# Last two layers in groups of four tiles, first transform by row tiles, and the gate logits of the last head pair one step later

## The chip, the cores and the metric

The kernel runs on one core of a Trainium2 chip. The metric is the device time of one launch in microseconds. In the profile PE is TensorE (PEld its weight loads), DVE is VectorE, ACT is ScalarE, POOL is GpSimd, and SP is the sync engine, which here only issues DMAs.

## What is computed

Three blocks in a row on 2 x 768 tokens of width 512, all in float32:

```python
# 1. attention: a window of +-15 keys plus 24 block summaries, 8 heads of 64
scores_all = np.concatenate([scores_l_m, scores_s], axis=-1)
a = softmax(scores_all);  out = a @ np.concatenate([v, v_sum], axis=2)
# 2. mixture of 8 experts, token by token; the expert is carried over while a local gate is >= 0.5
logits = x @ w_gate;  local_gate = sigmoid(x @ w_local)
e = argmax(logits[s]) if s == 0 or local_gate[s] < 0.5 else prev_e
out[s] = p[e] * (np.maximum(x[s] @ w1[e], 0) @ w2[e])
# 3. Fourier mixing over sequence and features, then two dense layers
u = x + np.real(fft2(x))
un = (u - mu) / np.sqrt(var + 1e-6)
y = u + np.maximum(un @ w_ch1, 0) @ w_ch2      # w_ch1 is 512 x 2048, w_ch2 2048 x 512
```

## The kernel before

Each engine has its own hand-written instruction stream, and semaphores tie them together. 128 tokens are a tile; there are 12 tiles, 6 of each batch (`ST` = 6, `NT` = 12).

**Attention** works through 8 pairs-of-heads steps in which `attend` handles the 6 tiles `t` of a pair: probabilities turned on PE (L1722), scores (L1713), values (L1736 to 1738). The tables `GATE_TURN`, `GATE_SUM` and `BEHIND` say beside which `(pair, t)` PE turns a tile's activations (`turn_gate`, L1745), ACT copies them to `mid` (`gate_rows`, L736), PE forms the 9 logits (`logits`, L1753) and DVE fetches them (`fetch_logits`, L990). In the last pair the logits of tile 6 stand at t = 3 and those of tiles 7 and 8 behind the values of t = 4 and 5; those of tiles 9 to 11 come after attention. Then PE turns the first 128 sorted rows (`turn_rows(0, 0)`, L1839), keeps busy with six unused matmuls (`unread`, L1882), and starts the first expert layer.

**Experts**: rows sorted by expert in steps of 128; every step has `first_layer` (L1851, 24 matmuls), `turn_rows` of the next step, `second_layer` of the previous one (L1876, 24 matmuls) and `turn_hidden` (L1863). Matmuls are exact splits of float32 in three products of rounded parts (high x high, low x high, high x low); ACT makes the high part and DVE subtracts for the low one (L1392). Four steps are written out and 18 stand in a loop with a test on the number in use (13 steps in this data); skipped ones cost only their tests. The last `second_layer(used - 1)` stands behind the loop. DVE scales the result (L1500), POOL scatters it to DRAM (`folded_y`, L593), SP waits for all of that and gathers the rows back (L492), one DMA for a row tile and its mirror.

**Transform**: DVE folds each gathered pair of row tiles in an even (L1528 to 1532) and an odd half (L1534 to 1543); `fold(b)` makes all three evens of a batch and then all three odds. PE first runs 40 unused matmuls (L2016), then `along_sequence(b)`: for each output chunk the sum over the three row tiles, two cosine chunks and one column (L1938 with a closing row L1940) and two sine chunks (L1951), in plain float32, which the trace counts as two matmuls each. `along_features` follows (L1962 to 1971), DVE and POOL add the results to natural and mirrored rows.

**Last two layers**: `GT` = 3 tiles form a group of `GN` = 384 tokens, in `GROUPS` = 4 groups: 0 and 2 are the natural halves of a batch, 1 and 3 the mirrored ones. A unit `F` is one of 16 chunks `f` of 128 hidden channels for one group: `first` is 12 matmuls of 384 columns into bank 2 or 3 (L1998), ACT takes relu (L885), DVE the low part (L1646), and `second` is 9 matmuls of 512 columns into banks 4 to 6 (L2011). PE does `first(F + 1)` ahead of `second(F)`. In every unit ACT and DVE also split the next 128 columns of `w_ch1` (L851, L1392) and rows of `w_ch2` (L856, L1392), since the weights are kept only as read. The activations of the next group are turned in four chunks during a group (`turn_centred`, L1988; `TURN_AT`). Mean and variance of all tiles are taken in group 0's units, and ACT takes the square root in unit 13 (`deviations`, L840). At the end of a group `finish` (L1614) scales the 3 banks and adds the residual; SP stores natural tiles (L505), POOL mirrored ones with an indirect DMA (L651). The four groups are a loop of two steps of two groups.

## Time and profile before

| | |
|---|---|
| time, three runs | 667.31 us median (666.71, 667.31, 671.98) |
| the profiled execution | 672.55 us, of which its span is 670.6 us |
| mean granted PE clock of it | 0.973 of full speed |
| busy | PE 625.5 us, DVE 364.0, ACT 270.8, POOL 129.2 |
| chain of work that ended last, by engine | PE 79%, DVE 6%, issue 4%, DMA 3%, ACT 3% |
| chain, costliest lines | L2011 20%, L1998 18%, L1876 10%, L1851 9% |
| stages of the span, by the timeline | attention to about 133 us, experts to 319.5, transform 319.5 to 384.9, last layers 384.9 to 659.8, stores and end to 670.6 |

The profile is of one execution of the program; its times are microseconds from the span's start. A chain row is a piece of work on the path that ended last; idle time of an engine off that path costs nothing.

### The profile page before, as it was taken

Reading aid. Unit: us, or ns where it says so; the run is one execution under the profiler, and the core shown is the slowest. Engines: PE = TensorE matmul, PEld = TensorE weight load, DVE = VectorE, ACT = ScalarE, POOL = GpSimd, SP = SyncE. Lnnn points to the kernel's source line nnn. Section 1 sums busy time; section 2 is a strip of 40 time slices with the busy share of each in tenths; the row PEclk is TensorE's granted clock in tenths of the full one; section 3 lists DMA queues with packets and bytes.
Section 4 is the critical chain, followed back from the end, with each engine's and each line's share of the span. In section 5 each row is a group of like instructions: output and inputs, shape, how many; then the busy total and the mean of one; then the engine's idle time right before and its main releaser. Section 6 shows DMA issues by size and latency. Waiting matters only on the chain.

```text
span 670.6 us, 11120 instructions
## 1 busy us (share of the span) xinstructions
PE 625.5 (93%) x3282; PEld 531.4 (79%) x3283; DVE 364.0 (54%) x956; ACT 270.8 (40%) x593; POOL 129.2 (19%) x155
## 2 busy tenths in 40 slices
PE   4799998899889999998899999999999999999993
PEld 3799998878667888886534589988999899989992
DVE  4788687568472585232451666655444544454441
ACT  3488775445132364111011534453443343433330
POOL 5566544203610010010000412030000310000001
PEclk9999999879999999998979999999999999999997
DMA  6958533694454455310503240001000100010001
GB/s 152 170 125 181 127 77 120 216 323 150 183 195 167 157 162 164 152 63 17 203 0 112 92 173 1 0 1 49 1 0 1 47 0 0 0 47 0 0 0 47
DMA packets 59300, 61.61 MB, mean 92 GB/s; under 512 B 42688, under 2 KB 42816, under 8 KB 58240
## 3 DMA queue, kind: packets, MB, share of 16 engines
q1 hardware_dynamic: 54384, 47.21, 24.0%
...
q14 instruction: 19, 0.16, 0.1%
...
## 4 chain that ended last, share of the span: by engine, by line
PE 79%; DVE 6%; issue 4%; DMA 3%; ACT 3%; SPq 1%; another core or an unknown queue 1%; POOL 1%; DVEq 0%; ACTq 0%; POOLq 0%
PE bank L2011 20%; PE bank L1998 18%; PE bank L1876 10%; PE bank L1851 9%; PE bank L1713 3%; PE bank L1938 2%; PE bank L1753 2%; PE bank L1722 2%; ACT arena L703 1%; PE bank L1839 1%; PE bank L1951 1%; PE bank L1863 1%; PE bank L1962 1%; PE bank L1736 1%; PE bank L1745 1%
## 5 line engine op out<-in xcount | busy, mean ns | idle before, releaser
L1998 PE MATMUL bank<-parts 128*128 128x384 f32 x768 | 146.1, 338 | 2.1 <-DVE parts L1392 2.1
L2011 PE MATMUL bank<-parts 128*128 128x512 f32 x576 | 143.8, 394 | 0.7 <-DVE parts L1646 0.3
L1392 DVE TENSOR_TENSOR parts<-arena,parts 128x512 fp32r<-128x512 f32 (+1 forms) x140 | 98.8, 737 | 83.0 <-ACT parts L856 77.9
L1998 PEld LDWEIGHTS bank<-parts 128*128 128x128 f32 x768 | 135.5, 188 | 7.1 <-DVE parts L1392 2.8
L2011 PEld LDWEIGHTS bank<-parts 128*128 128x128 f32 x576 | 106.7, 188 | 21.7 <-DVE mid L1614 1.3
L1851 PE MATMUL bank<-parts 128*128 128x512 f32 x312 | 77.8, 403 | 3.1 <-issue 2.3
L1876 PE MATMUL bank<-parts 128*128 128x512 f32 x312 | 76.2, 401 | 4.9 <-DVE parts L1392 4.5
L856 ACT ACTIVATE parts<-arena 128x512 fp32r<-128x512 f32 x64 | 40.4, 631 | 82.2 <-PE bank L2011 82.2
L1876 PEld LDWEIGHTS bank<-parts 128*128 128x128 f32 x312 | 58.8, 192 | 17.9 <-issue 3.6
L1851 PEld LDWEIGHTS bank<-parts 128*128 128x128 f32 x312 | 59.0, 193 | 16.5 <-issue 4.5
L1392 DVE TENSOR_TENSOR parts<-bank,parts 128x512 fp32r<-128x512 f32 (+1 forms) x56 | 35.1, 649 | 33.6 <-ACT parts L846 23.5
L885 ACT ACTIVATE parts<-bank 128x384 fp32r<-128x384 f32 x64 | 31.4, 491 | 53.7 <-PE bank L1998 53.7
L1646 DVE SCALAR_TENSOR_TENSOR parts<-bank,parts 128x384 fp32r<-128x384 f32 x64 | 35.6, 556 | 26.2 <-ACT parts L885 26.1
L703 ACT ACTIVATE arena<-arena,small 128x184 f32<-128x184 f32 x96 | 42.1, 440 | 15.3 <-DVE small L948 14.5
L651 POOL DMA_INDIRECT out<-mid,cst x6 | 6.1, 1020 | 203.0 <-DVE mid L1614 202.4
L1713 PE MATMUL bank<-arena 128*128 128x184 f32 x192 | 41.6, 344 | 1.8 <-ACT arena L683 1.3
L851 ACT ACTIVATE parts<-arena 128x512 fp32r<-128x512 f32 x64 | 39.5, 617 | 0.0
L593 POOL DMA_INDIRECT folded_y<-mid,dest_i x13 | 12.7, 978 | 129.6 <-DVE dest_i L1501 129.3
L549 POOL TENSOR_TENSOR mid<-mid 128x1024 f32<-128x1024 f32 (+3 forms) x28 | 33.7, 1205 | 12.5 <-DMA mid<-in_v 8.8
L795 ACT ACTIVATE parts<-bank 128x512 fp32r<-128x512 f32 x26 | 14.1, 594 | 51.4 <-PE bank L1863 39.2
L1713 PEld LDWEIGHTS bank<-arena 128*128 128x128 f32 x192 | 32.4, 207 | 3.0 <-ACT arena L683 1.7
L948 DVE CUSTOM_DVE_ANT_0 arena<-bank,cst 128x184 f32<-128x184 f32 x96 | 29.3, 342 | 9.7 <-PE bank L1713 8.8
...
## 6 DMA issues: line engine op xcount, KB each, us to landing
...
```

The costliest lines, as they stand in the source:

```text
L549: pool.tensor_tensor(blocks[:, par, 0:n], blocks[:, par, 0:n], blocks[:, par, n:2 * n], ALU.add).then_inc(halved, 1)
L703: last = act.activation(probs[:, t % 3, (2 * NSP - NS) * hh:(2 * NSP - NS) * hh + NS], masked[:, t % 3, hh, :], ACT.Exp, scale=-1.0, bias= ...
L851: act.activation(m1_hi[:, f % 2, :].rearrange("p (c n) -> p c n", c=DC), m1_raw[:, :, P * f:P * f + P], ACT.Copy).then_inc(m1h_ok, 1)
L856: act.activation(m2_hi[:, f % 2, :], m2_raw[:, f, :], ACT.Copy).then_inc(m2h_ok, 1)
L885: act.activation(g_hi[:, f % 2, :], bank[2 + f % 2][:, 0:GN], ACT.Relu).then_inc(ghi_ok, 1)
L1392: return dve.tensor_tensor(out, whole, upper.bitcast(F32), ALU.subtract)
L1646: dve.scalar_tensor_tensor(g_lo[:, f % 2, :], bank[2 + f % 2][:, 0:GN], 0.0, g_hi[:, f % 2, :].bitcast(F32), ALU.max, ALU.subtract).then_i ...
L1713: last = pe.matmul(S_BANK[t % 2][:, NS * hh:NS * hh + NS], qT[:, par, hh, P * t:P * t + P], k_win[:, par, t, keys], start=True, stop=True)
L1851: last = pe.matmul(bank[1 + half][:, :], x[:, r], w[:, c, f], start=(c == 0 and x is xT_hi and w is w1_hi), stop=(c == DC - 1 and w is w1_lo))
L1876: last = pe.matmul(bank[5][:, :], x[:, c, :], w[:, c // 2, f], start=(c == 0 and x is hT_hi and w is w2_hi), stop=(c == FC - 1 and w is w2 ...
L1998: last = pe.matmul(bank[2 + f % 2][:, 0:GN], w[:, f % 2, r], x[:, par, c, :], start=(c == 0 and w is m1_hi and x is cT_hi), stop=(c == DC ...
L2011: last = pe.matmul(bank[4 + t][:, :], x[:, f % 2, r], w[:, f % 2, :], start=(f == 0 and x is g_hi and w is m2_hi), stop=(f == MC - 1 and w ...
```

## The change

- **Groups of four.** `GT` becomes 4, so `GN` is 512 and there are 3 groups. The tiles are dealt out by a table `TILES`: group 0 takes tiles 0, 3, 1, 4 (two natural tiles of batch 0 and their mirrors), group 1 tiles 5, 9, 10, 11, group 2 tiles 2, 6, 7, 8. `first` has 12 matmuls of 512 columns and `second` 12 of 512, into banks 4 to 7; there are 48 units in place of 64, written out without loops and tests. The next group is turned at units 7, 9, 11, 13. ACT centres four tiles of group 0 and not three, two of them mirrored ones that POOL has to add first.
- **End of a group.** PE signals each finished tile of the last unit (`tile_ps`), and `finish` scales it then; `finish` stands ahead of the turned chunk and of `lower2`. The stores go tile by tile to SP (natural) and POOL (mirrored); the last group has natural tiles only. `out_sb` has its own place in `mid`.
- **Transform.** The first `along_sequence` goes by row tile: for tile j all cosine sums, then all sine sums, in five banks. `fold` makes even and odd of one tile before the next.
- **Last second layer** of the experts stands in the loop, under a test `used < n + 2`; the unused matmuls in front of the transform are 28 and not 40.
- **Gate.** In the last pair the logits are one step later: tile 6 at t = 4, tile 7 at t = 5, tiles 8 to 11 after attention; ACT's copies stay where they were (`GATE_COPY`). `turn_gate` of tiles 10 and 11 waits no longer for the copy ahead, the first sorted rows are turned between the logits of tiles 9 and 10, and the six unused matmuls are gone. DVE has the first two chunks of w1's low part ahead of the rows, and fetches two logits around the split of the rows.

```diff
-GT = 3
+GT = 4
-TURN_AT = {5: (0,), 7: (1,), 9: (2,), 11: (3,)}
+TURN_AT = {7: (0,), 9: (1,), 11: (2,), 13: (3,)}
+TILES = (0, KC, 1, KC + 1) + (KC + 2, ST + KC, ST + KC + 1, ST + KC + 2) + (2, ST, ST + 1, ST + 2)
...
-        BEHIND = {(PAIRS - 1, t): ST + t - 3 for t in (ST - 2, ST - 1)}
+        BEHIND = {(PAIRS - 1, t): ST + t - 4 for t in (ST - 2, ST - 1)}
...
+            for n in NATURAL:
+                sp.wait_ge(o_sb, n + 1 + GT)
+                b, c = TILES[n] // ST, TILES[n] % ST
+                sp.dma_start(out[b, P * c:P * c + P, :], out_sb[:, n % GT, :]).then_inc(natural_out[n % GT], 16)
...
+            fetch_logits(ST + 2)
+            lower_first(w1_lo, w1_raw, w1_hi, w1_hi_ok, w1_lo_ok, 0)
             fetch_logits(ST + 3)
-            lower_first(w1_lo, w1_raw, w1_hi, w1_hi_ok, w1_lo_ok, 0)
-            fetch_logits(ST + 4)
-            fetch_logits(ST + 5)
+            lower_first(w1_lo, w1_raw, w1_hi, w1_hi_ok, w1_lo_ok, 1)
             rows_landed(0)
             dve.tensor_copy(meta_next, xs(0)[:, DM:DM + 2]).then_inc(meta_in, 1)
+            fetch_logits(ST + 4)
             split_x(0)
-            for c in range(1, DC):
+            fetch_logits(ST + 5)
+            for c in range(2, DC):
...
             def fold(b):
                 for c in range(KC):
+                    fold_even(b, c)
+                    fold_odd(b, c)
...
             def finish(g):
-                dve.wait_ge(l2_ps, MC * (g + 1) + TWO)
                 dve.wait_ge(rstd_ok, 1)
                 for c in range(GT):
                     n = GT * g + c
-                    dve.wait_ge(o_free, n + 1)
+                    if c < GT - 1:
+                        dve.wait_ge(tile_ps, (GT - 1) * g + c + 1)
+                    else:
+                        dve.wait_ge(l2_ps, MC * (g + 1) + TWO)
+                    if g:
+                        dve.wait_ge(*stored(n - GT))
...
-            second_layer(used - 1)
+                        with pe.If(used < n + 2):
+                            second_layer(n)
...
+                if b == 0:
+                    for j in range(KC):
+                        pe.wait_ge(even_ok, j + 1)
+                        for o, r, free, n, done in to:
+                            cosines(o, r, j)
...
+                        pe.wait_ge(odd_ok, j + 1)
+                        for c in range(FD):
+                            last = sines(c, j)
...
-            for _ in range(40):
+            for _ in range(28):
                 pe.matmul(bank[7][:, :], xT_hi[:, 0:P], w1_hi[:, 0, 0:512], start=True, stop=True)
```

Two places of PE's order follow. The first is between attention and the experts. `128x9` rows are logits, `cst,x_all 128x128` rows with `xs_first0` turn the sorted rows, other such rows turn a tile for the gate, and `128x256` are the unused matmuls. Before:

```order
L1745 MATMUL bank<-cst,x_all 128x128 [waits xg_sb,att_out]
L1745 MATMUL bank<-cst,x_all 128x128 x3
L1753 MATMUL bank<-cst,mid 128x9 [waits xg_sb,lg_sb]
L1753 MATMUL bank<-cst,mid 128x9 x3
L1753 MATMUL bank<-cst,mid 128x9 [waits xg_sb,pT_sb]
L1753 MATMUL bank<-cst,mid 128x9 x3
L1839 MATMUL bank<-cst,x_all 128x128 [waits xs_first0,lg_sb]
L1839 MATMUL bank<-cst,x_all 128x128 x3
L1882 MATMUL bank<-cst 128x256 x3
L1843 TENSOR_LOAD table_i [waits lg_sb,table_ok]
```

The same place of the change:

```order
L1738 MATMUL bank<-cst,mid 128x9 [waits xg_sb,lg_sb]
L1738 MATMUL bank<-cst,mid 128x9 x3
L1730 MATMUL bank<-cst,x_all 128x128 [waits att_out]
L1730 MATMUL bank<-cst,x_all 128x128 x3
L1822 MATMUL bank<-cst,x_all 128x128 [waits xs_first0,lg_sb]
L1822 MATMUL bank<-cst,x_all 128x128 x3
L1738 MATMUL bank<-cst,mid 128x9 [waits xg_sb,pT_sb]
L1738 MATMUL bank<-cst,mid 128x9 x3
L1738 MATMUL bank<-cst,mid 128x9 [waits xg_sb]
L1738 MATMUL bank<-cst,mid 128x9 x3
L1826 TENSOR_LOAD table_i [waits lg_sb,table_ok]
```

The turned rows moved ahead of the last two sets of logits, the last gate tile is turned behind another set, and the unused matmuls are gone.

The second place is the start of the transform, PE: the unused matmuls, then batch 0 of `along_sequence`. `386` rows are cosine sums (`1x386` the single column, L1940 the closing row), `384` rows sine sums. Before:

```order
L2016 MATMUL bank<-parts 128x512 x40
L1938 MATMUL bank<-arena 128x386 [waits even_ok,yc_sb,tables_in]
L1938 MATMUL bank<-arena 128x386 [waits even_ok] x2
L1940 MATMUL bank<-cst,arena 128x386 [waits row_ok]
L1938 MATMUL bank<-arena 128x386 [waits even_ok,yc_sb]
L1938 MATMUL bank<-arena 128x386 [waits even_ok] x2
L1940 MATMUL bank<-cst,arena 128x386 [waits row_ok]
```

The change:

```order
L2023 MATMUL bank<-parts 128x512 x28
L1918 MATMUL bank<-arena 128x386 [waits ys_sb,z_sb,yc_sb,even_ok,tables_in]
L1918 MATMUL bank<-arena 128x386
L1918 MATMUL bank<-arena 1x386
L1921 MATMUL bank<-arena 128x384 [waits odd_ok]
L1921 MATMUL bank<-arena 128x384
L1918 MATMUL bank<-arena 128x386 [waits even_ok]
```

Five sums of the first row tile now stand ahead of the wait for the second tile; before, each chunk waited for all three tiles in turn.

## Rows read from the trace of the kernel before

**Rows 1.** The page, part 1: busy us (share of the span) x instructions

```profile
PE 625.5 (93%) x3282; PEld 531.4 (79%) x3283; DVE 364.0 (54%) x956; ACT 270.8 (40%) x593; POOL 129.2 (19%) x155
```

**Rows 2.** Chain that ended last (start, us, what): the last layers

```profile
400.34 2.10 PE bank L1998 x12
402.44 2.08 PE bank L2011 x9
...
655.67 4.14 PE bank L2011 x18
```

**Rows 3.** Timeline (start, us, engine line op, [idle before <-releaser]), the last layers

```profile
438.86 0.49 PE L1988 MATMUL bank<-cst,mid 128*128 128x128 f32 x3
...
448.52 2.37 PE L1998 MATMUL bank<-parts 128*128 128x384 f32 x12 [0.79 <-DVE parts L1392]
...
459.53 2.34 PE L2011 MATMUL bank<-parts 128*128 128x512 f32 x9 [0.26 <-DVE mid L1614]
```

**Rows 4.** Timeline of the end

```profile
659.99 2.07 DVE L1614 SCALAR_TENSOR_TENSOR mid<-bank,small,x_all 128x512 f32<-128x512 f32 x3 [3.20 <-PE bank L2011]
...
663.66 0.96 POOL L651 DMA_INDIRECT out<-mid,cst  x1 [0.30 <-issue]
```

**Rows 5.** DMA issues from 590 us on (count, KB each, us to landing)

```profile
out<-mid SPq DMA_DIRECT2D x3, 256.0 KB, 2.1
out<-mid,cst POOLq DMA_INDIRECT x3, 2.7
```

**Rows 6.** Timeline, end of the experts and start of the transform

```profile
310.16 1.29 DVE L1392 TENSOR_TENSOR parts<-bank,parts 128x512 fp32r<-128x512 f32 x2
...
312.09 7.37 PE L1876 MATMUL bank<-parts 128*128 128x512 f32 x24 [2.82 <-DVE parts L1392]
...
319.29 9.23 PE L2016 MATMUL bank<-parts 128*128 128x512 f32 x40
...
327.34 0.69 DVE L1528 TENSOR_TENSOR mid<-x_all 128x512 f32<-128x512 f32 x1 [6.89 <-DMA x_all<-folded_y]
...
328.77 0.89 PE L1938 MATMUL bank<-arena 128*128 128x386 f32 x2 [0.25 <-DVE arena L1532]
...
331.77 0.69 DVE L1528 TENSOR_TENSOR mid<-x_all 128x512 f32<-128x512 f32 x1 [1.80 <-DMA x_all<-folded_y]
```

**Rows 7.** Windows: length, busy PE, PEld, DVE, ACT, POOL, granted clock, DMA share, GB/s

```profile
313.60:317.00 3.40, 3.40 (x10) 2.66 (x9) 0.00 (x0) 0.00 (x0) 0.00 (x0) 0.50 0.00 0
334.10:344.30 10.20, 9.99 (x15) 3.43 (x16) 9.92 (x35) 0.98 (x2) 0.00 (x0) 0.50 0.02 7
344.50:384.00 39.50, 38.29 (x136) 19.85 (x134) 11.04 (x26) 12.21 (x28) 7.48 (x10) 1.00 0.22 80
```

**Rows 8.** Timeline, between attention and the experts

```profile
125.61 1.03 PE L1753 MATMUL bank<-cst,mid 128*128 128x9 f32 x8 [1.03 <-ACT mid L736]
...
131.05 3.67 SPq L445 DMA_DIRECT2D x_all<-sorted_x  x4
...
135.90 3.23 PE L1753 MATMUL bank<-cst,mid 128*128 128x9 f32 x16
...
142.00 4.53 PEld L1851 LDWEIGHTS bank<-parts 128*128 128x128 f32 x18
```

**Rows 9.** Timeline, start of the last layers

```profile
376.51 0.72 ACT L836 ACTIVATE mid<-x_all,small 128x512 f32<-128x512 f32 x1
...
384.88 4.44 PE L1998 MATMUL bank<-parts 128*128 128x384 f32 x24 [1.31 <-DVE parts L1392]
```

**Rows 10.** Chain, `along_sequence` of batch 1: its first and last piece

```profile
349.86 1.95 PE bank L1938 x6
...
358.41 4.09 PE bank L1951 x12
```

**Rows 11.** DMA issues from 117 to 145 us: the sorted rows

```profile
x_all<-sorted_x SPq DMA_DIRECT2D x4, 258.0 KB, 3.2
```

**Rows 12.** Chain, experts: a piece that no engine's row explains

```profile
178.73 4.40 another core or an unknown queue
```

332 lines of the change are left out of this document (153 added, 179 removed).

## The prediction

> **What bounds the kernel now.** I read the page first: PE is busy for 93% of the span [rows 1], so what counts is how fast PE gets through its work and where it is idle or slow. Next the chain of work that ended last: from 384.9 us to 659.8 it is almost only PE, 2.10 us for a `first` (12 matmuls of 384 columns) and 2.08 for a `second` (9 of 512), one behind the other [rows 2]. The timeline of that stretch shows what breaks it [rows 3], and that of the end shows 10.8 us between the last matmul (655.67 + 4.14 = 659.81) and the span's end, of which the last finish, the last indirect DMA and its landing are the larger part [rows 4, 5]. Then the passages between stages: from the last expert step to the transform PE waits, runs unused matmuls and waits again [rows 6], and the windows show PE at a granted clock of 0.50 (1.2 GHz and not 2.4) in two stretches there [rows 7]. The passage from attention to the experts has the same pattern [rows 8].
>
> **The sum** is made against the profiled execution, 672.55 us, whose span is 670.6; about 2 us lie outside the span and stay. That execution is 5.2 us above the median of the three runs, 667.31, and close to their highest, 671.98. One of the stretches at half clock lasts 10.2 us [rows 7], which costs up to 5.1 us. That is the size of the step between the runs, so I take it that the median runs lack most of it. The change takes this stretch away, so the sum should hold for its median as it stands.
>
> *1. Last layers, -3.9.* There are 48 units in place of 64. One matmul of 512 columns takes 2.08 / 9 = 0.231 us, one of 384 2.10 / 12 = 0.175 [rows 2]. Before: 64 x 4.18 = 267.5. After: 48 x 24 x 0.231 = 266.1. Gain 1.4: the columns stay the same, and only a small fixed part of 192 fewer matmuls goes. Turning the next groups takes 12 insertions of 3 transposes now, about 0.33 us each (an x3 row of 0.49 whose first 0.16 overlaps [rows 3]), and 8 of 4 afterwards at 0.44: 0.5. The square root makes PE wait 0.79 once [rows 3], since ACT's table loads are longer than the room in a 4.18 us unit; a 5.54 us unit has 1.4 more, so the wait should go: 0.8. Each of three later groups starts with 0.26 of waiting for `finish` [rows 3]. `finish` will start tile by tile, a whole `first` (2.8 us) ahead of the bank's next use: 0.8. What is left of the stretch, 274.9 - 267.5 - 4.0 - 0.8 - 0.8 = 1.8, should shrink by a quarter, 0.4. ACT and DVE have three operations of 512 columns each in a unit, at 0.7 us like others of that size [rows 6, 9]: 2.1 us in 5.5, so they stay hidden.
> A rule of the Trainium skill ("TensorE: Matmul & The Clock Gate", section "Wait — 56ns, not 53.3ns?") speaks against even the 1.4: at the full clock matmuls start N / 2.4 GHz + about 2.5 ns apart. By it 192 fewer matmuls would be worth 0.5 and this part 3.0. The rows say 7 ns, and I go by the rows.
>
> *2. Start of the last layers, +1.1.* ACT now centres four tiles. A tile is three instructions, the last of them 0.72 us [rows 9], about 1.5 in all. It delays the weight split and the two copies behind it; the copies and low parts of the turned chunks are 512 and not 384 columns wide, on the path three times or so by 0.15. PE's other work hides part of this; already now PE waits 1.31 for DVE here [rows 9]. Bounds: 0 (all hidden) and +2.0 (none).
>
> *3. End, -3.4.* From the last matmul on, three tiles are scaled (2.07 us), and three indirect DMAs go out one behind the other; the last is issued 663.66 - 659.81 = 3.85 us after it and lands 2.7 later: 6.55 [rows 4, 5]. After: the last tile is scaled 0.2 after the last matmul in 0.75, and a direct DMA lands 2.1 later [rows 4, 5]: 3.1. Bounds -2.5 to -3.8.
>
> *4. Last second layer, -2.1.* The first half of its input is ready at 310.16 + 0.65 = 310.8, but PE starts only at 312.09 [rows 6], because its sequencer has to step over nine unused loop steps first. In the loop it starts at about 311.0: 1.1. It then runs at half clock for 3.4 us [rows 7], behind 2.8 us of idle PE. With 1.7 idle I expect the clock to stay: 1.7 more. Against that the stepping now comes behind it, so the unused matmuls start about 2.3 us late (12 fewer of them, 2.8 us, fit this), and a clock that falls there could end them too late: +0.7. Bounds 0 and -2.8. The extra test in each loop step lies behind the 8 transposes of `turn_hidden`, and PE shows no gap there now; uncovered it would cost some 0.1 each, 0.9.
>
> *5. Transform of batch 0, -8.0.* From 328.77 to 349.86 is 21.1 us; batch 1 with the same matmuls runs from 349.86 to 362.50, 12.6 us, at full clock [rows 7, 10]. The difference is waiting for row tiles (the third arrives at 331.77 [rows 6]) and 10.2 us at half clock [rows 7]. By row tile PE has 3.5 us of work (12.6 less the closing rows, in three) for each fold pair of about 2.5 us on DVE: DVE needs 1.3 us from a tile's arrival to its even half and 1.2 for the odd one, 0.7 more once for the single row, so even halves come at 0, 3.1 and 5.6 us after the first, and PE asks for them at 0, 3.5 and 7.0. It should run through without a wait: -8.5. Batch 1's last fold is ready 13.7 us after the start, and PE asks for it at about 14; I leave 0.5 for that. Bounds: -8.5, and -3.4 if the clock is low for as long as before.
>
> *6. Gate and first expert step, -4.0.* Before: 1.03 us of waiting for ACT's copy at 125.61, the last two logits at half clock in 3.2 us, then the turned rows and six unused matmuls, and the expert matmuls' weights from 142.0 [rows 8]. After: nothing waits for that copy, but one set of logits more (0.9 us) comes behind attention, and the rows cannot be turned before they land: issued from 131.05, 3.2 us [rows 8, 11], so 134.3. PE gets there at about 134 to 135. Then 1.7 us of logits hide ACT's copy and DVE's split of the rows (0.7 each, like others of 512 columns [rows 6, 9]), so expert matmuls start at about 137, 5 us earlier, perhaps with up to 3.4 us at half clock as now. DVE has two of w1's four chunks ready by then, and the other two are made behind them. I expect 4.6 at the end of this step and carry 4.0 through the experts, since what waits there (low parts, table, scatter) hangs on the same engines and moves with them. Bounds: -1.0, if the rows or w1's parts are late or a later load absorbs it, and -6.0.
>
> Sum: -3.9 + 1.1 - 3.4 - 2.1 - 8.0 - 4.0 = -20.3, so 672.55 - 20.3 = 652.2 us. That is 15.1 us, 2.3%, under the median before.
>
> **The rivals.**
> - *The clock stays low in the transform.* For: before the first sum PE will be idle for a while twice, and at 334.1 to 344.3 the clock was low although PE was busy for 9.99 of 10.20 us [rows 7], so this kind of matmul does not bring it back soon. Against: it fell while PE stood waiting for the third row tile, which came to DVE at 331.77 [rows 6], and row tiles fill that wait. Price 5.1: 657.3. Chance 0.17.
> - *The gain of part 6 is absorbed* by the loads of the next experts or by the row load: 652.2 + 4.0 = 656.2. For: once in the experts all engines stand for 4.4 us behind something that is no engine's work [rows 12]. Against: loads are issued when DVE has released the buffer, so they move too. Chance 0.12; both of these, 661.3, 0.05.
> - *The median runs' 5.2 us lie elsewhere,* in something the change leaves alone: then the median is 652.2 - 5.2 = 647.0. Against: the size fits the half clock. Chance 0.08.
> - *Slower.* The last layers are written out in full, 48 units and no loop. If an engine had to wait for its program there, and a wait cost what the 4.40 us row costs [rows 12], four such waits would bring it back to the median before (15.1 / 4.4 = 3.4), and from five on it is slower by over 1%: 652.2 + 5 x 4.4 = 674.2. Against: before, 32 units stand in a row in the loop and run twice, and the spacing of 2.10 and 2.08 holds from end to end [rows 2]; 1344 matmuls are issued then and 1152 afterwards. Chance 0.03.
> The Trainium skill ("Runtime: NRT & Kernel Launch", "Terms") says that an engine's instruction memory is refilled in blocks of 16 KiB. No row here ties a stall to it; it would be the mechanism of this rival.
> - *It does less than it says in several parts* (skipped steps cost nothing, start bound at its worst, end at its least): -20.3 + 2.1 + 0.9 + 0.9 + 3 = -13.4, 659.2. Chance 0.05.
>
> **How the numbers follow.** The forecast, 652.2, has the remaining chance of 0.5, with its own range 648 to 656. The range 646 to 660 takes in the first two rivals, the one below and the last; outside are both together and the slower one, and a tail of each, below 0.2. A difference of 1% (6.7 us) is about what a measurement of this kernel can tell from none. Faster by over 1% is under 660.6: 0.86, that is all but the double miss, the slower case and tails of the others; within 1% 0.1; slower 0.04.
>
> **What would show it.** In the profile after: rows of 12 matmuls of 512 columns in 2.77 us on both lines of the last layers, no PE wait at the square root, under 272 us from the first `first` to the last matmul; 7.3 us from there to the span's end; batch 0 of the transform within 13.5 us at a granted clock of 1.00; the last second layer starting within 0.3 us of the first half of its input; expert matmuls starting 5 us earlier than 142.0. Half clock in a dense stretch of the transform, PE waits in the middle of the last layers, or an expert stage that ends less than 4 us earlier would show the steps that fail.

## The result and the profile after

| | before | after |
|---|---|---|
| time, median of four runs each | 669.52 us (666.71 to 671.98) | 641.63 us (639.09 to 642.69) |
| the profiled execution, and its span | 672.55, 670.6 | 639.09, 637.0 |
| its mean granted PE clock | 0.973 | 0.991 |
| PE busy | 625.5 us | 604.4 us |
| last layers: first `first` to last matmul | 274.9 us | 265.3 us |
| last matmul to the span's end | 10.8 us | 3.7 us |

After takes 0.958 of the time before (0.952 to 0.964). The forecast was 652.2 with a range of 646 to 660: the sign was right, the gain about ten microseconds too small. In one experiment further down, second_old, one execution of four took 873.27 us at a mean clock of 0.658, and its median leaves that one out.

The mean clock of before holds an idle tail. Behind its last matmul PE does nothing, and for the last 8.6 us of the span the clock stands at 0.50 (window of before: length, busy PE, PEld, DVE, ACT, POOL, clock, DMA share, GB/s). That lowers the mean by 0.006 and costs no matmul any time; after has almost no such tail.

```profile
662.00:670.60 8.60, 0.00 (x0) 0.00 (x0) 0.06 (x1) 0.00 (x0) 2.01 (x3) 0.50 0.23 91
```

The page after, the busy time of PE and its two costliest lines, which answer to [rows 1] and to the two lines of [rows 2]:

```profile
PE 604.4 (95%) x3072; PEld 497.5 (78%) x3073; DVE 339.9 (53%) x902; ACT 248.6 (39%) x542; POOL 127.1 (20%) x154
L2003 PE MATMUL bank<-parts 128*128 128x512 f32 x576 | 139.4, 391 | 1.6 <-DVE parts L1387 1.6
L2016 PE MATMUL bank<-parts 128*128 128x512 f32 x576 | 138.2, 389 | 0.0
```

In the 576 matmuls of each line PE stands idle 1.6 us ahead of the first line and never ahead of the second: the waits for the square root and for `finish` in [rows 3] are gone. The chain that ended last (start, us, what) gives the length of 12 matmuls of 512 columns, against 2.10 and 2.08 in [rows 2]:

```profile
373.72 2.72 PE bank L2016 x12
376.44 2.72 PE bank L2003 x12
```

The timeline of the passage from the experts to the transform, which answers to [rows 6]. L1859 is the last second layer, L2023 the 28 unused matmuls, L1918 and L1921 the cosine and sine sums:

```profile
304.08 5.74 PE L1859 MATMUL bank<-parts 128*128 128x512 f32 x24 [1.74 <-DVE parts L1387]
310.69 6.62 PE L2023 MATMUL bank<-parts 128*128 128x512 f32 x28 [0.88 <-issue]
319.23 2.27 PE L1918 MATMUL bank<-arena 128*128 128x386 f32 x6 [1.92 <-DVE arena L1528]
321.44 1.56 PE L1921 MATMUL bank<-arena 128*128 128x384 f32 x4
```

Batch 0's sums run without a wait. The windows (length, busy PE, PEld, DVE, ACT, POOL, granted clock, DMA share, GB/s) show full clock for them, where [rows 7] had 10.2 us at 0.50, and the last layers at full clock as before:

```profile
319.23:332.26 13.03, 13.03 (x37) 5.53 (x38) 12.65 (x43) 1.96 (x4) 0.00 (x0) 1.00 0.38 144
367.98:633.33 265.35, 265.35 (x1184) 219.27 (x1184) 117.92 (x199) 87.81 (x152) 21.90 (x16) 1.00 0.05 20
```

The timeline at the passage to the experts, against [rows 8]. L1738 are logits, L1822 the turned rows, L1834 the first expert matmuls:

```profile
133.48 0.60 PE L1822 MATMUL bank<-cst,x_all 128*128 128x128 f32 x4
133.92 1.85 PE L1738 MATMUL bank<-cst,mid 128*128 128x9 f32 x16
140.06 0.82 PE L1748 MATMUL bank<-cst,small 128*8 128x128 f32 x6
```

The 18 expert matmuls between the last two of these rows start at 135.82. And the end, against [rows 4]: the four scaled tiles and their direct stores, with nothing from POOL:

```profile
631.39 2.73 DVE L1620 SCALAR_TENSOR_TENSOR mid<-bank,small,x_all 128x512 f32<-128x512 f32 x4 [2.15 <-PE bank L2016]
632.17 2.31 SPq L515 DMA_DIRECT2D out<-mid  x4
```

Term by term, from the two profiled executions. Each measured number is the difference of one stretch, and together they make the 33.6 us between the spans:

| stretch (before; after) | forecast | measured |
|---|---|---|
| 6: up to the last second layer, without the test's 1.1 | -4.0 | -6.9, of which -1.2 stands before the first changed instruction (the same scores start at 110.23 and at 109.02) |
| 4: last but one second layer to the first sum of the transform | -2.1 | -2.6 |
| 5: transform of batch 0 (328.77 to 349.86; 319.23 to 332.26) | -8.0 | -8.1 |
| 2: batch 1 to the first `first` (349.86 to 384.88; 332.26 to 367.98) | +1.1 | +0.7 |
| 1: last layers (384.88 to 659.81; 367.98 to 633.33) | -3.9 | -9.6 |
| 3: last matmul to the span's end | -3.4 | -7.1 |

So the two terms that missed by most are the ones about matmuls that only change their shape and about a transfer that changes its queue. The profiled execution of before is 3.0 us above its median and that of after 2.5 below its own, which is why the medians differ by 27.9 and not by 33.5.

### The profile page after: what moved, and what is told of

The parts are those of the page before. It is cut to its first block, busy times and chain, and to the rows that moved or that the text cites. A ratio compares the mean times of both kernels' runs of the same rounds, so it can differ in the third digit from the quotient of the medians.

```text
span 637.0 us, 10225 instructions
## 1 busy us (share of the span) xinstructions
PE 604.4 (95%) x3072; PEld 497.5 (78%) x3073; DVE 339.9 (53%) x902; ACT 248.6 (39%) x542; POOL 127.1 (20%) x154
## 4 chain that ended last, share of the span: by engine, by line
PE 78%; DVE 6%; issue 5%; DMA 4%; ACT 2%; SPq 2%; another core or an unknown queue 1%; POOL 1%; DVEq 0%; ACTq 0%; POOLq 0%
PE bank L2003 21%; PE bank L2016 20%; PE bank L1859 10%; PE bank L1834 9%; PE bank L1697 2%; PE bank L1918 2%; PE bank L1706 1%; ACT arena L706 1%; PE bank L1921 1%; PE bank L1967 1%; DVE parts L1387 1%; PE bank L1846 1%; DMA sorted_x<-zero_row,small 1%; PE bank L1976 1%
## 5 line engine op out<-in xcount | busy, mean ns | idle before, releaser
L2003 PE MATMUL bank<-parts 128*128 128x512 f32 x576 | 139.4, 391 | 1.6 <-DVE parts L1387 1.6
L2016 PE MATMUL bank<-parts 128*128 128x512 f32 x576 | 138.2, 389 | 0.0
L2003 PEld LDWEIGHTS bank<-parts 128*128 128x128 f32 x576 | 107.4, 188 | 24.0 <-DVE parts L1387 1.8
L2016 PEld LDWEIGHTS bank<-parts 128*128 128x128 f32 x576 | 108.1, 188 | 22.5
L1387 DVE TENSOR_TENSOR parts<-arena,parts 128x512 fp32r<-128x512 f32 (+1 forms) x108 | 77.0, 744 | 79.5 <-ACT parts L863 75.8
L1834 PE MATMUL bank<-parts 128*128 128x512 f32 x312 | 77.2, 400 | 2.7 <-issue 1.8
L1859 PE MATMUL bank<-parts 128*128 128x512 f32 x312 | 74.5, 394 | 4.1 <-DVE parts L1387 3.8
L1834 PEld LDWEIGHTS bank<-parts 128*128 128x128 f32 x312 | 58.2, 191 | 16.3 <-issue 4.6
L1859 PEld LDWEIGHTS bank<-parts 128*128 128x128 f32 x312 | 57.6, 188 | 16.6 <-issue 2.5
L863 ACT ACTIVATE parts<-arena 128x512 fp32r<-128x512 f32 x48 | 30.3, 631 | 82.9 <-PE bank L2016 82.9
L1645 DVE SCALAR_TENSOR_TENSOR parts<-bank,parts 128x512 fp32r<-128x512 f32 x48 | 33.2, 691 | 48.2 <-ACT parts L888 48.2
L888 ACT ACTIVATE parts<-bank 128x512 fp32r<-128x512 f32 x48 | 28.7, 598 | 69.3 <-PE bank L2003 67.8
L1387 DVE TENSOR_TENSOR parts<-bank,parts 128x512 fp32r<-128x512 f32 x52 | 34.4, 686 | 27.7 <-ACT parts L853 20.7
L706 ACT ACTIVATE arena<-arena,small 128x184 f32<-128x184 f32 x96 | 42.1, 440 | 16.1 <-DVE small L943 15.3
L798 ACT ACTIVATE parts<-bank 128x512 fp32r<-128x512 f32 x26 | 14.1, 594 | 52.5 <-PE bank L1846 40.4
L1497 DVE TENSOR_SCALAR mid<-bank,small 128x512 f32<-128x512 f32 x13 | 9.7, 750 | 40.6 <-PE bank L1859 34.5
L858 ACT ACTIVATE parts<-arena 128x512 fp32r<-128x512 f32 x48 | 29.7, 618 | 0.0
```

Source lines behind the costliest of these rows:

```text
L706: last = act.activation(probs[:, t % 3, (2 * NSP - NS) * hh:(2 * NSP - NS) * hh + NS], masked[:, t % 3, hh, :], ACT.Exp, scale=-1.0, bias= ...
L858: act.activation(m1_hi[:, f % 2, :].rearrange("p (c n) -> p c n", c=DC), m1_raw[:, :, P * f:P * f + P], ACT.Copy).then_inc(m1h_ok, 1)
L863: act.activation(m2_hi[:, f % 2, :], m2_raw[:, f, :], ACT.Copy).then_inc(m2h_ok, 1)
L1387: return dve.tensor_tensor(out, whole, upper.bitcast(F32), ALU.subtract)
L1645: dve.scalar_tensor_tensor(g_lo[:, f % 2, :], bank[2 + f % 2][:, 0:GN], 0.0, g_hi[:, f % 2, :].bitcast(F32), ALU.max, ALU.subtract).then_i ...
L1834: last = pe.matmul(bank[1 + half][:, :], x[:, r], w[:, c, f], start=(c == 0 and x is xT_hi and w is w1_hi), stop=(c == DC - 1 and w is w1_lo))
```

## The experiments

Times are medians. The kernel before was run beside each of four groups, each on a chip of its own, and its median depends on the chip: 668.4 us beside u3_unrolled, pool_end, seq_old and gate_old; 659.4 beside g2_pairs, second_old, second_seq_old and pool_one; 668.8 beside after_again, gate_alone, ladder and pool_plain; 659.9 beside layers_alone, transform_alone, fill36 and after_third. After itself was run beside only two of them (668.8 and 659.9). So kernels are compared within a group where that is possible. A comparison with after's 641.6 reaches across groups and is good to a few microseconds only; it is marked "about". g2_pairs, ladder and pool_plain are one execution each, and every profile is of one execution.

### Where the last layers' 9.6 us come from

**u3_unrolled**: before, with the loops and tests of the last layers written out, groups of three.

```diff
-            with pe.Fori(0, GROUPS // 2) as step:
+            for step in range(GROUPS // 2):
-                                with pe.If(more):
+                                if more:
```

> The kernel before with its last layers written out: the four groups of three stay, only the two-step loop and its tests on ACT, DVE and PE are gone, so every wait is on a constant. The last layers took 274.9 us before and 265.4 in the change, 9.6 less where 3.9 was forecast. Theory A (the loop's register work costs some 0.04 us per group of matmuls): a first of 12x384 falls from 2.10 to about 2.08 and a second of 9x512 from 2.08 to 2.04 us, the stretch by 3 to 4.5 us, the time by 3 to 4.5 us. Theory B (a fixed cost per matmul group, whatever its size, which only fewer groups lessen): 2.10 and 2.08 stay, the time moves by less than 1 us.

Measured: 665.1 us beside 668.4, ratio 0.997 (0.994 to 1.001). The chain (54 pieces of L2011 at 2.08, 46 of L1998 at 2.10 among its rows) is that of [rows 2]:

```profile
392.17 2.10 PE bank L1998 x12
394.27 2.08 PE bank L2011 x9
```

So loops and tests cost the matmuls nothing. From the first `first` to the last matmul are 273.6 us (385.28 to 658.92) and 274.9 in before: PE's wait of 0.79 us at the square root [rows 3] is not there in this run, which is most of the difference. The 3.3 us between the medians are not clear of noise. The other eight of the 9.6 us are not the loop's.

**g2_pairs**: after, with groups of two tiles, so 96 units of 12 matmuls of 256 columns and 6 of 512.

```diff
-GT = 4
+GT = 2
-NORMALISED = (1, 2, 0)
+NORMALISED = (1, 2, 3, 4, 5, 0)
```

> After with groups of two tiles: 6 groups, 96 units, each of 12 matmuls of 256 columns and 6 of 512. It gives a fourth and a fifth shape beside 12x384 (2.10 us), 9x512 (2.08) and 12x512 (2.72). Theory A, a fixed cost of about 0.16 us for each group of matmuls between two waits and nothing for a single matmul (2.10 = 12x0.160+0.18, 2.08 = 9x0.2133+0.16, 2.72 = 12x0.2133+0.16): the first line shows 12x0.1067+0.16 = 1.44 us, the second 6x0.2133+0.16 = 1.44 us, a unit 2.88, and 96 units 276.5 us in place of 261.0, so the program takes about 15 us more than after (about 656). Theory B, the forecast's cost for each matmul (0.231 us for 512 columns, 0.175 for 384, so about 0.0155 above the columns): the first line shows 12x0.122 = 1.47 us, the second 6x0.231 = 1.39 us, a unit 2.86. The second line tells them apart: 1.44 or 1.39. ACT and DVE, which split 1024 columns of weights and one hidden chunk in a unit, have about 2.3 us of work in it and could become the bound (theory C): then PE shows idle time before each group, and a unit is over 2.95 us.

Measured: 651.7 us (one execution). The chain:

```profile
411.19 1.39 PE bank L2019 x6
412.80 1.43 PE bank L2006 x12
```

1.39 on the second line is theory B's number, 1.43 on the first is nearer theory A's 1.44 than B's 1.47. A unit is 2.82 us, less than either said (2.88 and 2.86). No fixed cost per group explains that, and no single cost per matmul taken from the 9x512 row does. I had been fitting two unknowns to rows that hold a third, and measured the matmuls by themselves:

**ladder**: after, with rows of matmuls behind the last one, in the kernel's own shapes, each row on its own line. Its time, 753.0 us, holds these extra rows.

```diff
+            for i in range(4):
+                for o, w, x, k in like_first(512, i % 2, False):
+                    pe.matmul(o, w, x, **k)
...
+            for i in range(6):
+                for o, w, x, k in like_second(3, True):
+                    last = pe.matmul(o, w, x, **k)
+                last.then_inc(tile_ps, 1)
```

> After with ten rows of matmuls added behind the last one (nothing else works then; outputs unchanged), in groups as in the last layers: 4 groups of 12 into one bank of 512, of 384 and of 256 columns without waits; 4 of 12x512 over four banks without waits; then with a wait ahead and a signal behind every group 4 of 12x512 in one bank, 4 of 12x512 over four banks, 6 of 9x512 over three, 8 of 6x512 over two, 4 of 12x384, and 4 times 12x384 and 9x512 in turn, each row on its own line. Theory A, 0.16 us belongs to each group between two waits and nothing to a matmul: without waits 48 matmuls take 10.2, 7.7 and 5.1 us, with them 10.9 (12x512), 10.9 (over four banks), 12.5 for 54 (9x512), 11.5 for 48 (6x512). Theory B, the cost is per matmul (0.0133 at 512 columns by 2.72/12, up to 0.018 by 2.08/9): waits make no difference, all of 48x512 take 10.9 and 48x384 8.4. Theory C, it is neither but the other engines' traffic beside them (ACT and DVE read the same banks and write the weights in the real units): here, with nothing beside, each takes only its columns, 10.2, 7.7 and 5.1, with waits too.

Measured, from start to start of the rows of the timeline (L2068, L2071, L2074: 48 matmuls of 512, 384 and 256 columns without waits; L2088: 54 in groups of nine with waits; L2100 and L2103: the unit of before, 12x384 and 9x512 in turn):

```profile
633.80 11.04 PE L2068 MATMUL bank<-parts 128*128 128x512 f32 x48
644.68 8.51 PE L2071 MATMUL bank<-parts 128*128 128x384 f32 x48
653.03 5.91 PE L2074 MATMUL bank<-parts 128*128 128x256 f32 x48
658.77 11.07 PE L2077 MATMUL bank<-parts 128*128 128x512 f32 x48
691.44 12.40 PE L2088 MATMUL bank<-parts 128*128 128x512 f32 x54
724.99 2.24 PE L2103 MATMUL bank<-parts 128*128 128x512 f32 x9
727.07 2.27 PE L2100 MATMUL bank<-parts 128*128 128x384 f32 x12
729.17 2.24 PE L2103 MATMUL bank<-parts 128*128 128x512 f32 x9
```

One matmul of 512 columns takes 10.88 / 48 = 0.2267 us, of 384 8.35 / 48 = 0.1740, of 256 5.74 / 48 = 0.1196. With a wait and a signal around every group it is the same: the next row starts at 703.68, and 12.24 / 54 = 0.2267 for groups of nine. Theory A falls, theory C too (nothing works beside these rows), and B holds at the low end of its price: 0.013 us for each matmul above columns / 2.4 GHz. Where widths alternate, something is added: a pair of 12x384 and 9x512 should take 12 x 0.1740 + 9 x 0.2267 = 4.13 us and takes 4.18 (724.99 to 729.17), 0.05 more for a change there and back. In the kernel before it is 64 pairs of 4.185 and so 3.6 us. After has one width only, and its 48 units are 48 x 24 x 0.2267 = 261.1 us of the 265.35 in its window; the rest is the turned groups and the start. So of the 6.7 us that the matmuls of the last layers gave (267.8 less 261.1), 3.6 are the changes of width and 3.1 the 192 matmuls fewer. I have no row that says what the change of width does inside PE.

### What stands behind the last transfer

**pool_end**: after, with the last group's four stores by POOL's indirect transfers, as in before.

```diff
-NATURAL = [n for n in range(NT) if TILES[n] % ST < KC]
+NATURAL = [n for n in range(NT - GT) if TILES[n] % ST < KC]
```

> The changed kernel with the four stores of the last group made by POOL's indirect DMA and not by SP. From the last matmul to the span's end it was 10.8 us before and 3.7 in the change, 7.1 less where 3.4 was forecast. Theory A (only the issue and landing of the last stores count): +2.5 to +3.5 us against the change. Theory B (an indirect DMA of POOL late in the program also lengthens what comes after the last landing): +6 to +8 us, with 3 us or more in which no engine and no DMA works.

Measured: 647.0 us beside 668.4, ratio 0.969 (0.961 to 0.977). The last store on the timeline, in a span of 645.9 us (POOL's four stand 1.26 apart):

```profile
638.41 0.96 POOL L658 DMA_INDIRECT out<-mid,cst  x1 [0.30 <-issue]
```

From its issue to the span's end are 7.5 us, of which the landing is 2.7. From the last matmul to the end are 10.4 us and not 3.7: theory B. Of the 6.7 us more than in after, some 2.4 are the later landing; in the rest the profile shows no engine and no store at work.

**pool_one**: after, with only the first of the last four stores by POOL.

```diff
-NATURAL = [n for n in range(NT) if TILES[n] % ST < KC]
+NATURAL = [n for n in range(NT) if TILES[n] % ST < KC and n != NT - GT]
```

> After with one of the last four stores, the first, issued by POOL as an indirect transfer, and the other three by SP as they are. With all four by POOL the span ended 7.5 us behind the last issue, 2.7 of them to landing. Theory A, each POOL transfer holds the end until about 7.5 us behind its issue: the issue stands at about 632.3, so the span ends at about 640, 2.5 to 3 us later than after. Theory B, only what lands last counts: the POOL transfer lands at about 635.5, ahead of SP's last, and the span ends at about 637 as after. Theory C, a fixed 4 us at the end once POOL has issued any transfer behind the last matmuls, counted from the last landing of all: the span ends at about 641.

**pool_plain**: the same store, as a plain transfer of POOL.

```diff
+                if n == NT - GT:
+                    pool.dma_start(out[TILES[n] // ST, P * (TILES[n] % ST):P * (TILES[n] % ST) + P, :], out_sb[:, n % GT, :]).then_inc(mirrored_out[n % GT], 16)
+                    continue
```

> After with the first of the last four stores by POOL as a plain transfer, the other three by SP. With the indirect transfer there the span ended 7.5 us behind its issue (629.59 to 637.1), as it did with four of them (638.41 to 645.9) against about 2.5 us behind SP's last issue in after. Theory A, any transfer that POOL issues itself holds the end for 7.5 us from its issue: the span ends about 7.5 us behind it, 3 us later behind the last matmul than in after (6.6 against 3.7 us). Theory B, only the indirect one does: the span ends 3.7 us behind the last matmul.

Measured: 639.3 us beside 659.4, ratio 0.970 (0.967 to 0.973), and 641.6 (one execution) on another chip. The last rows of both timelines (spans 637.1 and 639.4):

```profile
629.59 0.96 POOL L658 DMA_INDIRECT out<-mid,cst  x1 [78.84 <-DVE mid L1620]
630.00 1.65 SPq L515 DMA_DIRECT2D out<-mid  x3
```

```profile
632.52 0.60 POOL L659 DMA_DIRECT2D out<-mid  x1 [78.86 <-DVE mid L1623]
632.90 1.67 SPq L515 DMA_DIRECT2D out<-mid  x3
```

7.5 us from POOL's issue to the end again, although SP's last landing comes later than POOL's, and 6.9 us for the plain transfer. Behind SP's last issue alone the span ended after 2.5 us (634.48 to 637.0). So it is neither the number of POOL's transfers nor their indirect addresses. From the last matmul to the end are 6.6 us in pool_one and 6.0 in pool_plain, against 3.7 in after: theory A in both, exact in pool_one and 0.6 us under its 6.6 in pool_plain. Theory C of pool_one, 4 us behind the last landing of all, falls: SP's last store lands 2.8 us behind its issue at 631.65, which leaves 2.7. Why POOL's transfer holds the end is not shown. Whichever engine is last, the program does not end sooner than about 7 us behind the last transfer that POOL issues itself. The kernel before fits: its last issue stands at 663.66 [rows 4], its end at 670.6, 6.9 later.

### The transform and the last second layer

**seq_old**: after, with the transform's sums by output chunk and all evens before the odds, as in before; the 28 unused matmuls stay.

```diff
                 for c in range(KC):
                     fold_even(b, c)
+                for c in range(KC):
                     fold_odd(b, c)
...
-                if b == 0:
+                if False:
```

> The changed kernel with the first transform in the old order: all even halves before the odd ones on DVE, one output chunk after the other on PE; 28 unused matmuls stay. Theory A (waits for row tiles and the half clock that they bring): +7 to +9 us, batch 0 in about 21 us with some 10 us at a granted clock of 0.50. Theory B (most of the 17.6 - 9.6 = 8 us came from the clock's luck and not from the order): the clock stays at 1.00 and the loss is 3 to 4 us.

Measured: 645.6 us beside 668.4, ratio 0.968 (0.960 to 0.978), about 4 more than after's 641.6. The profile is of its fastest execution (640.7 us, mean clock 0.995); the other three took 644.0 to 647.8 at 0.983 to 0.992. The timeline shows the waits for the row tiles back, at full clock:

```profile
319.60 0.92 PE L1919 MATMUL bank<-arena 128*128 128x386 f32 x2 [0.36 <-DVE arena L1528]
321.50 0.92 PE L1919 MATMUL bank<-arena 128*128 128x386 f32 x2 [0.98 <-DVE arena L1528]
323.08 0.91 PE L1925 MATMUL bank<-cst,arena 1*128 1x386 f32 x2 [0.67 <-DVE arena L1540]
```

```profile
318.35:333.66 15.31, 13.30 (x36) 5.38 (x37) 13.35 (x44) 1.96 (x4) 0.00 (x0) 1.00 0.32 122
```

Batch 0 takes 15.3 us, against 13.0 in after and 21.1 in before. So the order is worth 2.3 us at full clock, and the other 5.8 of the term are not the order's alone. The rest of the 4 us goes with the lower clock of the other three executions. By its time and this window it is theory B; those executions show that the clock doesn't always stay full.

**second_old**: after, with the last second layer behind the loop.

```diff
-                        with pe.If(used < n + 2):
-                            second_layer(n)
+            second_layer(used - 1)
```

> After with the last second layer back behind the loop (part 4 alone undone; 28 unused matmuls stay). Theory A, its tests cost what the chain showed before, 0 to 2.8 us, and the half clock of 3.4 us that stood over it before comes back with the idle time: the last second layer begins 1 us later, takes 7.4 us in place of 5.7, and the program is 2 to 3 us slower than after, and more if the half clock reaches the transform again (5 us). Theory B, the place costs only the idle time on PE (1.1 us in after against before): the last second layer begins about 1 us later, takes 5.7 us, the clock stays at full speed through the transform, and the program is within 1.5 us of after.

Measured: 637.5 us (637.5 to 643.5) beside 659.4, ratio 0.972 (0.966 to 0.978). Its timeline:

```profile
301.02 5.73 PE L1859 MATMUL bank<-parts 128*128 128x512 f32 x24 [2.80 <-DVE parts L1387]
306.59 6.51 PE L2022 MATMUL bank<-parts 128*128 128x512 f32 x28
```

From the last but one second layer to this one are 9.39 us, and 8.33 in after (295.75 to 304.08): the place in the loop is worth 1.07 us. It runs at full clock here although PE was idle for 2.8 us. In time that is theory B. But the clock does not stay full through the transform, as B had it; it falls in the first sums:

```profile
317.15:320.50 3.35, 3.35 (x6) 0.92 (x5) 3.25 (x12) 0.00 (x0) 0.00 (x0) 0.50 1.01 387
```

**second_seq_old**: the edits of `seq_old` and `second_old` together.

> After with parts 4 and 5 undone together: last second layer behind the loop, and the transform's first sums by chunk as before. With the transform's order alone undone, batch 0 took 15.3 us and the clock stayed full. Theory A, the two half-clock stretches of before in the transform (10.2 us at half clock, about 5 us) came from the two parts together, by the longer idle stretches in a row: the clock falls at or behind the last second layer again and once more in the transform, batch 0 takes 17 to 21 us, and the program is 8 to 11 us slower than after. Theory B, they came from elsewhere (from when this stretch is reached, which the gate part moved: with the gate part undone the clock fell in the transform, at 323.9 and 337.4): the clock stays full, and the program is 4 to 5 us slower than after, the sum of the two parts alone.

Measured: 645.4 us beside 659.4, ratio 0.980 (0.977 to 0.983), with `pool_one` at 639.3 on the same chip, which itself stands about 2.9 above after. That is 9 us more than after, and a stretch at half clock as long as that of [rows 7] is back, in the sums of the same batch:

```profile
315.25:325.50 10.25, 9.37 (x14) 3.35 (x12) 8.81 (x30) 0.49 (x1) 0.00 (x0) 0.50 0.45 171
```

Theory A in size: apart, the two edits cost about 1 and 4 us, together about 9. The clock did not fall at the last second layer (5.73 us), but in the sums, and the surplus is half clock; the five executions have a mean clock of 0.976 to 0.987.

### The gate part, and whether the parts add up

**gate_old**: after, with the gate part undone (tables, banks, the order of logits and rows, six unused matmuls).

```diff
-            logits(ST + 4)
-            logits(ST + 5)
+            logits(ST + 5)
+            pe.wait_ge(lg_sb, ST + 4)
+            turn_rows(0, 0)
+            unread(3)
             pe.wait_ge(table_ok, 1)
```

> The changed kernel with the gate part undone: logits of tiles 6 to 8 inside attention, six unused matmuls, the sorted rows turned behind all logits, DVE's old order. Theory A (the order there is worth what the traces show, expert matmuls at 135.8 and not 142.1 us): +4.5 to +6.5 us, expert matmuls from about 141 us. Theory B (an early start is absorbed in the experts by loads and tables): expert matmuls start 5 us later, but the loop of the experts less than 3 us later, and the time grows by less than 3 us.

Measured: 648.0 us beside 668.4, ratio 0.972 (0.964 to 0.980), about 6.4 more than after's 641.6. That is theory A's time, but not its start: the expert matmuls begin 2.7 us later than in after (135.82), where both theories had five or more, and the last but one second layer 4.1 later (299.89 against 295.75).

```profile
138.48 4.97 PE L1833 MATMUL bank<-parts 128*128 128x512 f32 x18
```

Two stretches of half clock in a transform that is after's are of the size of the rest. They are no mark of this edit, since after itself shows two in the profile of after_again:

```profile
323.90:327.20 3.30, 3.30 (x6) 0.62 (x5) 3.15 (x13) 0.00 (x0) 0.00 (x0) 0.50 0.98 355
337.40:340.90 3.50, 3.50 (x7) 1.89 (x6) 0.00 (x0) 0.93 (x2) 0.00 (x0) 0.51 0.00 0
```

**gate_alone**: before, with the gate part alone, the same lines the other way round.

```diff
-            turn_rows(0, 0)
-            unread(3)
+            turn_rows(0, 0)
+            pe.wait_ge(pT_sb, ST * PAIRS + TWO)
+            logits(ST + 4)
+            logits(ST + 5)
             pe.wait_ge(table_ok, 1)
```

> Before with the gate part alone (logits of the last pair a step later, expert rows turned between logits). Undone in after, this part cost 6.4 us. Theory A, it is worth the same by itself: the first matmuls of the experts begin 6 us earlier than in before (142.1 there), and the program is 4 to 7 us faster. Theory B, the gain depends on the clock, which was half for 3.5 us over the first expert matmuls of before and again later: the stretch of half clock is only moved to another place, the experts begin 6 us earlier but the program is only 1 to 3 us faster, since the old transform's stretches of half clock stay.

Measured: 666.5 us beside 668.8, ratio 0.998 (0.995 to 1.001), so the 2.3 us are not clear of noise. The expert matmuls begin 6.7 us earlier than in before (142.08):

```profile
135.38 4.38 PE L1853 MATMUL bank<-parts 128*128 128x512 f32 x18
```

and they keep that lead up to the last second layer (305.49 against 312.09), but the program gains 2.3 us and no more. About half of the lead is clock: before stands at half clock from 136.1 us until past its first expert matmul, so that its 16 logits take 3.23 us [rows 8] and 1.85 here. But half clock stands elsewhere as before, in the experts and in the transform:

```profile
175.25:182.25 7.00, 6.41 (x15) 4.56 (x15) 5.18 (x16) 5.17 (x7) 1.17 (x1) 0.51 0.15 59
325.75:332.25 6.50, 6.12 (x9) 2.72 (x10) 6.33 (x24) 0.49 (x1) 0.00 (x0) 0.50 0.23 89
```

The mean granted clock of its runs is 0.977, no higher than before's 0.979. Theory B in size: what the part saves ahead of the experts, the program gives back behind them, in stretches of half clock.

There is a second reason why the part has no fixed worth. In all ten profiles on chips where before takes 668 us or more, DVE stands for 1.9 to 2.6 us in the last head pair, behind something that the profile finds on no engine of this core ("remote"). In the eight profiles on the other two chips it never does. The row of u3_unrolled:

```profile
115.96 0.29 DVE L978 TENSOR_TENSOR x_all<-bank,small 128x128 f32<-128x128 f32 x1 [2.55 <-remote]
```

With that wait the old gate part starts the expert matmuls at 142.08, 141.01 and 138.48 (before, u3_unrolled, gate_old), and the new one at 134.1 to 135.8. Without it they are 135.58 and 137.16 (layers_alone, transform_alone) against 133.7 to 134.5. So ahead of the experts the gate part is worth 3 to 8 us on one kind of chip and 1 to 3 on the other. What DVE waits for is not shown.

**transform_alone**: before, with parts 4 and 5. **layers_alone**: before, with parts 1 to 3.

```diff
-            second_layer(used - 1)
+                        with pe.If(used < n + 2):
+                            second_layer(n)
...
-            for _ in range(40):
+            for _ in range(28):
```

```diff
-GT = 3
+GT = 4
-TURN_AT = {5: (0,), 7: (1,), 9: (2,), 11: (3,)}
+TURN_AT = {7: (0,), 9: (1,), 11: (2,), 13: (3,)}
```

The second takes with it the tiles' table, `finish` and the order of the stores.

> Before with the last second layer in the loop, 28 unused matmuls and the transform by row tiles alone (parts 4 and 5). Undone in after they cost 9 us together (on one chip), most of it half clock. Theory A, they are worth the same by themselves: 7 to 9 us faster than before, the mean clock rises from 0.979 to about 0.987 and over. Theory B, as with the gate part (6.4 us when undone in after, 2.3 when done alone in before) the stretches of half clock only move: 1.1 us for the test in the loop and 2.4 for the order of the sums remain, 3 to 4 us in all, at a clock that stays below 0.983.

> Before with the last two layers and the end of after alone (parts 1 to 3); gate, last second layer, unused matmuls and transform as in before. Theory A, the parts add up: last layers 9.6 us shorter, their start 0.7 later, the end 7.1 shorter, so the program is 16 us faster than before (668.8 becomes 653), its mean granted clock stays at 0.979. Theory B, they don't, and more of what after gained belongs to the last layers (the clock, say): the program is over 20 us faster.

Measured, beside 659.9: transform_alone 650.7, ratio 0.988 (0.982 to 0.994); layers_alone 644.2, ratio 0.978 (0.974 to 0.983). The windows of batch 0's sums in the two:

```profile
316.31:329.18 12.87, 12.87 (x37) 5.37 (x37) 12.52 (x42) 1.91 (x4) 0.00 (x0) 1.00 0.40 150
```

```profile
317.92:333.83 15.91, 13.30 (x37) 5.38 (x38) 13.34 (x44) 1.96 (x4) 0.00 (x0) 1.00 0.32 120
```

Parts 4 and 5 give 9.1 us by themselves (4 to 12 by the interval of the ratio), and the median of the mean clock rises from 0.979 to 0.989: theory A, though 4 us, theory B's, is not ruled out. Parts 1 to 3 give 15.7 us, of the 16.0 that the two profiles had (9.6 + 7.1 - 0.7): theory A in time. Their mean clock rises too, to a median of 0.986 where theory A had it stay, and the missing idle tail of before (0.006) is just that much. On this chip the parts add up to 24.8 us without the gate part, and after is 24.2 faster than before: here the gate part adds nothing that can be seen. With before at 668.8 after is 28.6 faster.

The second window says more. layers_alone has before's passage and before's order of the sums, and yet its sums run at full clock in this execution, its fastest (640.9 us at 0.992; the others 643.6 to 645.6 at 0.984 to 0.987). Half clock in the transform, over all eighteen profiled executions: with the old order of the sums 10.2 us (before), 13.6 (u3_unrolled), 10.2 (second_seq_old), 6.8 (gate_alone), each in one stretch, and twice none (seq_old, layers_alone); with the new order none in four (after, pool_end, ladder, transform_alone), 3.4 in five (second_old, pool_one, pool_plain, fill36, after_third) and two stretches of 3.4 in three (gate_old, g2_pairs, after_again). So the old passage is more at risk, and one profile does not say what a kernel has.

**fill36**: after, with 36 unused matmuls ahead of the transform. **after_again**, **after_third**: after once more in each group.

```diff
-            for _ in range(28):
+            for _ in range(36):
```

> After with 36 unused matmuls in front of the transform and not 28: 8 more take 8 x 0.2267 = 1.8 us and fill the 1.92 us for which PE waits there. Theory A, the stretches of half clock seen in the transform of after (two of 3.3 us in one profile, none in another) follow from that idle time: they go, the mean clock is 0.993 or more and the program is 1 to 3 us faster than after. Theory B, they come from what lies further back, or the eight matmuls delay the first sum where the fold is earlier: within 1 us of after.

> After as it is, timed a second time beside the kernel before. The kernel before has come out at 669.5, 668.4 and 659.4 us (medians) on different chips. Theory A, a chip that is faster for before is faster for after by as much, and what is off in the forecast is in the parts: after's ratio stays at 0.958, so after shows about 640 beside 668 and about 632 beside 659. Theory B, after has little of what varies (two stretches of half clock in its transform, 10.2 us at half speed in the profiled execution of before, which the forecast took away): after stays at 638 to 643 whatever before shows, and the ratio goes to 0.97 on a chip where before is at 659.

> After as it is, on the same chip as the three others, to compare them with: 638 to 643 us.

Measured: fill36 636.7 us (635.9 to 637.9), after_third 635.7 (634.7 to 639.0), after_again 640.1 beside 668.8, ratio 0.959 (0.955 to 0.963). In fill36 the idle time ahead of the first sum is gone, and yet the clock falls eleven microseconds later, with PE busy without a gap since 305.84:

```profile
305.84 8.43 PE L2023 MATMUL bank<-parts 128*128 128x512 f32 x36 [0.88 <-issue]
314.26 2.28 PE L1918 MATMUL bank<-arena 128*128 128x386 f32 x6
```

```profile
325.75:329.00 3.25, 3.25 (x6) 1.85 (x6) 2.12 (x7) 1.26 (x3) 0.00 (x0) 0.50 0.00 0
```

Theory B of that run: this stretch does not come from the idle time right ahead of the transform. It stands at about the same place in after_third, and in after_again there are two (322.00 and 335.50), while the first profile of after has none. What decides between one, two and none stays open. For the ratio, neither theory of after_again holds on both chips: 0.959 on one as at first, 0.966 (0.961 to 0.971) on the other, where before is 9 us faster and after 4.4, so that after_third lies below the 638 to 643 expected of it. DVE's wait in the last head pair goes with most of the 4.6 us between the two: the profiles with it start the experts some 4 us later under the old gate part, and under after's less than one. The 4.4 that both kernels gain are not explained by it; most of them stand in the experts (135.82 to 304.08 in after, 134.48 to 298.87 in after_third).

## Why the prediction was off

**Term 1, the last layers, failed in its price.** The step is "one matmul of 512 columns takes 2.08 / 9 = 0.231 us". It takes 0.2267, and that is the 5.0 us between the forecast's 266.1 and 261.1. What the row of nine holds beyond the matmuls is the change of width, 0.05 us in each unit, and dividing it by nine turned it into a property of every matmul, to be paid again 1152 times in a kernel that no longer changes width. A row of before had the right price: the 40 unused matmuls of [rows 6], one width and one line, take 9.23 us, which with the same tail as the ladder's rows (11.04 shown for 10.88) is 9.07 / 40 = 0.2267. The small terms (transposes, square root, `finish`, rest; 2.5) came to 2.9, and 0.8 of that, the square root's wait, goes with the loop alone (u3_unrolled).

The Trainium skill ("TensorE: Matmul & The Clock Gate", section "Wait — 56ns, not 53.3ns?") has N / 2.4 GHz + about 2.5 ns from start to start, which the prediction weighed and left. The ladder agrees with its form, a slope of columns / 2.4 GHz and one fixed cost per matmul that waits do not change, and not with its size: 0.2267 - 0.2133 is 13 ns, with a new weight load ahead of each matmul.

**Term 2** was right in size (+1.1, +0.7).

**Term 3, the end, failed in what it held fixed.** Scaling, issue and landing were forecast at 3.1 us from the last matmul on, and that agrees, since the whole span ends 3.7 us behind it. The step that failed is the one that isn't in the sum: 10.8 us less 6.55 left 4.2 us in which nothing works [rows 4, 5], and the prediction carried them over unchanged ("7.3 us from there to the span's end"). They belong to POOL's transfer, and with them gone the end is 7.1 us shorter and not 3.4. pool_one shows it best, where a POOL transfer is issued and lands before SP's last and still holds the end.

**Term 4** was right for its first half (1.1; 1.07 measured with and without). Its second half, 1.7 for the clock, came true in this profile (5.74 and not 7.37 us). Behind 1.7 us of idle PE the last second layer ran at full clock in all twelve profiles that have it in the loop. Behind 2.8 us it ran at half clock in four (before, u3_unrolled, gate_alone, layers_alone) and at full clock in two (second_old, second_seq_old). So the longer idle time goes with the half clock, but does not alone decide it.

**Term 5** hit its number by luck, for both profiled executions helped. The order alone is worth 2.3 to 3.0 us at full clock (15.3 and 15.9 against 13.0 and 12.9). The other 5 us are half clock that before's execution had (10.2 us) and after's had not, while after has 3.4 us of it in after_third and 6.8 in after_again, and layers_alone, with before's transform, has none. The reading that the clock fell while PE waited for the third row tile is wrong: PE was back at work at 333.12 and the clock fell at 334.1, and seq_old and layers_alone have that wait (0.98 and 1.59 us) and full clock. A stretch of more than 3.4 us stands only where parts 4 and 5 are both old, in four profiles of five. The rival that the clock stays low in the transform, given 0.17, is thus half true of after: 3.4 us or more in eight of the twelve profiles that have the new order.

**Term 6** was right at the start of the experts: 6.3 us earlier, less the 1.2 that stand before any changed instruction, are the 5 that were forecast. (That row starts at 107.9 to 110.2 in the eighteen profiles, latest in before.) Carried on it was too low by about 1.7 (5.7 against 4.0), since none was absorbed on the way to the last second layer, so the rival on absorption falls as it was put. But the forecast read the wait for ACT's copy at 125.61 as the kernel's own, while it comes with a wait of DVE that two of the chips do not show, and done alone the part brings 2.3 us, which noise does not tell from none.

**The median.** The guess was that the median runs lack most of the long stretch at half clock. In size that holds: the mean granted clock of before is 0.979 in the median of every group and 0.973 in the profiled execution, which makes some 8 us less of half clock and 4 us of time, near the 5.2 that it was to explain. Within a group the time follows the clock: beside u3_unrolled before took 660.9 us at 0.995, 665.5 at 0.984 and 671.6 at 0.976. That the missing stretch is the one in the transform is not shown. Nor does the guess explain the miss: against the profiled execution of after the sum is off by 13.1 us, against the median by 10.6. From chip to chip the clock explains nothing, since before has 0.979 at 668.4 us and at 659.4.

The rival of program waits is without support: in the written-out layers of after a group of 12 matmuls takes 2.72 us in 83 of its chain rows and never more than 2.77.
